# An attention scan's opening: products of the first eight groups split in two, evicted in pairs, and the work around them moved

## The reference

```python
k_n = k / (np.linalg.norm(k, axis=-1, keepdims=True) + 1e-06)
state = np.zeros((B, H, D, D))
for t in range(S):                       # B, H, S, D = 4, 8, 768, 48
    kt, vt, bt = k_n[:, :, t], v[:, :, t], beta[:, :, t, None]
    y[:, :, t] = q[:, :, t] @ state
    state = state + bt * outer(kt, vt - kt @ state)
x = y as (3072 tokens, 384)
h = x @ w_in;  g = (a0 + a1 h + a2 h^2 + a3 h^3) / (1 + |b0| |h| + |b1| h^2 + 1e-06);  x = g @ w_out
h = x @ w2_in; g = relu(h)^2;  out = g @ w2_out          # both 384 -> 2048 -> 384
```

## Time and profile before

| | |
|---|---|
| median of 3 runs (lowest, highest) | 1108.83 us (1108.4, 1108.87) |
| the profiled execution | 1109.15 us, of which the profile's span is 1107.4 us |
| PE, PEld busy | 98%, 85% of the span |
| DVE, ACT, POOL busy | 61%, 59%, 45% |
| granted TensorE clock, mean | 0.997 |
| bytes moved | 74.42 MB, 67 GB/s over the span |

### The profile page before, as it was taken

The page is one execution under the profiler, slowest core; times in us unless marked ns, Lnnn a source line. Parts: engine busy times, 40 slices in busy tenths (PEclk is TensorE's granted clock), DMA queues, the critical chain, the costliest instruction groups (busy, mean ns, idle before and its releaser), DMA issues.

```text
span 1107.4 us, 18346 instructions
## 1 busy us (share of the span) xinstructions
PE 1089.6 (98%) x6370; PEld 940.5 (85%) x6370; DVE 673.2 (61%) x1087; ACT 651.6 (59%) x1277; POOL 502.2 (45%) x807
## 2 busy tenths in 40 slices
PE   8799999999999999999999999999999999999998
PEld 6599999999987888888888888888888888888887
DVE  6976554445459988788887889854343333334332
ACT  5576666555669777877878778653333333333322
POOL 5284888682039878777787778400000000000000
PEclk9999999999999999999999999999999999999999
DMA  9958787566421010100101012140100101010000
GB/s 198 186 103 195 157 180 146 118 148 174 107 73 58 30 57 1 57 1 1 57 1 57 1 44 71 43 129 1 57 1 21 37 1 57 0 57 1 1 29 29
DMA packets 174043, 74.42 MB, mean 67 GB/s; under 512 B 136000, under 2 KB 161728, under 8 KB 172992
## 3 DMA queue, kind: packets, MB, share of 16 engines
q1 hardware_dynamic: 164352, 68.54, 25.5%
q10 hardware_dynamic: 9600, 4.72, 1.8%
HBM read 52.27 MB, written 20.71 MB: 66 GB/s over the span
## 4 chain that ended last, share of the span: by engine, by line
PE 85%; POOL 6%; DVE 4%; issue 2%; SPq 1%; DMA 1%; ACT 0%; ACTq 0%; POOLq 0%
PE ps L1192 12%; PE ps L1194 11%; PE ps L1193 11%; PE ps L1178 11%; PE ps L1180 11%; PE ps L1179 11%; POOL shared L444 3%; POOL scan_x L437 3%; PE ps L548 2%; PE ps L592 2%; PE ps L578 2%; PE ps L595 2%; PE ps L558 2%; PE ps L564 2%; PE ps L525 1%
## 5 line engine op out<-in xcount | busy, mean ns | idle before, releaser
L1178 PE MATMUL ps<-x_split,weights 128*128 128x512 f32 x576 | 224.8, 390 | 1.7 <-DVE g_lo L1337 1.2
L1192 PE MATMUL ps<-g_hi,weights 128*128 128x512 f32 x576 | 224.2, 389 | 0.1
L1180 PE MATMUL ps<-x_split,weights 128*128 128x512 f32 x576 | 224.2, 389 | 0.0
L1179 PE MATMUL ps<-x_split,weights 128*128 128x512 f32 x576 | 224.1, 389 | 0.0
L1193 PE MATMUL ps<-g_lo,weights 128*128 128x512 f32 x576 | 224.1, 389 | 0.0
L1194 PE MATMUL ps<-g_hi,weights 128*128 128x512 f32 x576 | 224.1, 389 | 0.0
L1347 DVE TENSOR_TENSOR common<-common 128x512 f32<-128x512 f32 x96 | 66.4, 692 | 135.0 <-ACT common L1251 133.5
L1257 ACT ACTIVATE g_hi<-common 128x512 fp32r<-128x512 f32 x96 | 60.9, 634 | 141.7 <-PE ps L1194 137.2
L1178 PEld LDWEIGHTS ps<-x_split,weights 128*128 128x128 f32 x576 | 108.1, 188 | 25.2 <-DVE g_lo L1337 2.3
L1410 POOL TENSOR_TENSOR common<-common,g_hi 128x512 f32<-128x512 f32 x96 | 124.2, 1294 | 8.7 <-DVE g_hi L1325 8.7
L1403 POOL TENSOR_TENSOR common<-common 128x512 f32<-128x512 f32 x96 | 124.5, 1297 | 8.0
(11 more groups left out here) (118 smaller groups left out, 1904.5 us busy)
## 6 DMA issues: line engine op xcount, KB each, us to landing
scan_late<-kq_in SPq DMA_DIRECT2D x10, 768.0 KB, 6.5
scan_late<-kq_in SPq DMA_DIRECT2D x16, 384.0 KB, 4.3
shared<-w_in SPq DMA_DIRECT2D x32, 192.0 KB, 2.5
shared<-w_out SPq DMA_DIRECT2D x32, 192.0 KB, 2.6
x_first<-y_t ACTq DMA_DIRECT2D x24, 192.0 KB, 2.7
shared<-x_first SPq DMA_DIRECT2D x6, 768.0 KB, 5.8
x_second<-shared SPq DMA_DIRECT2D x6, 768.0 KB, 4.2
shared<-x_second SPq DMA_DIRECT2D x6, 768.0 KB, 5.9
```

The source lines that it names most:

```text
L1178: pe.matmul(bank(n), lo, x_hi[:, slot, k, :], start=(k == 0), stop=False)
L1179: pe.matmul(bank(n), hi, x_lo[:, slot, k, :], start=False, stop=False)
L1180: mm = pe.matmul(bank(n), hi, x_hi[:, slot, k, :], start=False, stop=(k == KT - 1))
L1192: pe.matmul(ps_y[m], lo, g_hi[:, d, :], start=(f == 0), stop=False)
```

## The change

Six edits. (1) For groups 0 to 7 TensorE makes N alone (`first_n(g)`, a moving operand of 64 columns), and after all eight it makes P (`first_p(g)`, again 64 columns, with the same stationary operand loaded anew, each after `n_first` and after the queries' own load `first_q_loaded`). (2) DVE takes N of two groups in one go (`take_first_pair`: three instructions of 64 x 256 elements for two groups); the eight PSUM banks become one tensor so that an access can span two of them. (3) `load_first` loads only keys, in halves of the former size; the queries of quads 0 and 1 follow in two loads of their own. (4) `k_diag` gets two more slots (`k_diag_aside`, memory that the state uses later), so `spread_keys(2)` and `(3)` wait for no products; `spread_keys(4)` and `(5)` move to behind the second and the fourth `copy_products`, which now waits for `np_done`. A second place for squares (`k_sq_aside`) lets quads 2 and 3 be squared without the wait for the sum just before. (5) The scaling of v of quad 0 by its norms moves from one POOL instruction (L458) to 16 ACT activations of 48 columns, placed behind `squares(4)`. (6) In SP's steps, `load_k(h)` for h >= 9 moves ahead of `store_n`.

```diff
+        z_room = late.take(8 * PAIRS * D)
+        k_sq_aside = z_room[:, 0:QP * D].rearrange("p (q d) -> p q d", q=QP)
+        k_diag_aside = common.ap[0:D2, common.at:common.at + 16 * PAIRS * BL].rearrange(
+            "r (s g f h t) -> r s g f h t", s=2, g=2, h=2, t=BL)
...
+        def squares_of(h):
+            return k_sq_aside if h in (1, 3) else k_sq
+        def diag_of(j):
+            return k_diag_aside[:, j - 2] if j in (2, 3) else k_diag[:, j % 2]
...
-                sp.dma_start(kq[:, j // 2, :, pair], kq_in[:, j // 2, :, pair]).then_inc(first_loaded[j], 16)
+                sp.dma_start(kq[:, j // 2, 0, pair], kq_in[:, j // 2, 0, pair]).then_inc(first_loaded[j], 16)
+            def load_first_q(h):
+                sp.dma_start(kq[:, h, 1], kq_in[:, h, 1]).then_inc(first_q_loaded[h], 16)
...
+            for h in range(2):
+                load_first_q(h)
             load_kq_aside(2)
...
+                for h in range(9, QUADS):
+                    if n == 4 * h - 26:
+                        load_k(h)
                 for h in range(4, QUADS):
                     if n == step_of_quad(h):
                         store_n(h)
...
-                for h in range(8, QUADS):
-                    if n == 4 * h - 26:
-                        load_k(h)
+                if n == 4 * 8 - 26:
+                    load_k(8)
...
-            scale_first_v()        # POOL
...
+            def first_n(g):
+                pe.wait_ge(k_diag_ready, g // 2 + 1)
+                keys_loaded(pe, g // 2)
+                for p in range(PAIRS):
+                    mm = pe.matmul(np_bank(g)[:, p, 0:C],
+                                   diag_of(g // 2)[:, g % 2, 2 * p:2 * p + 2].rearrange("r f h t -> r (f h t)"),
+                                   keys_of(g // 4)[:, 0, g % 4 * PAIRS + p, :], start=True, stop=True)
+                mm.then_inc(n_done, 1)
+            def first_p(g):
+                pe.wait_ge(n_first, g + 1)
+                pe.wait_ge(first_q_loaded[g // 4], 16)
+                for p in range(PAIRS):
+                    mm = pe.matmul(np_bank(g)[:, p, C:2 * C],
+                                   diag_of(g // 2)[:, g % 2, 2 * p:2 * p + 2].rearrange("r f h t -> r (f h t)"),
+                                   keys_of(g // 4)[:, 1, g % 4 * PAIRS + p, :], start=True, stop=True)
+                mm.then_inc(np_done, 1)
...
-            for g in range(UPFRONT):
+            for g in range(FIRST):
+                first_n(g)
+            for g in range(FIRST):
+                first_p(g)
+            for g in range(FIRST, UPFRONT):
                 products(g)
...
-                if h > 0:
+                if h in (2, 3):
+                    act.wait_ge(sum_ready, h - 1)
+                elif h > 3:
                     act.wait_ge(sum_ready, h)
...
-                if j >= 2:
-                    act.wait_ge(np_done, 2 * j - 2)
+                if j >= 4:
+                    act.wait_ge(np_done, 2 * j - (6 if j < 6 else 2))
...
+            def scale_first_v():
+                act.wait_ge(v_loaded[0], 16)
+                values = ring(0)[:, :, :, 0:D].rearrange("r g p d -> r (g p) d")
+                for q in range(QP):
+                    mm = act.activation(values[:, q, :], values[:, q, :], ACT.Copy, scale=norm[:, q:q + 1])
+                mm.then_inc(v_by_act, 1)
             def copy_products(g):
-                if g < FIRST:
-                    act.wait_ge(n_first, g + 1)
+                act.wait_ge(np_done, g + 1)
...
             for g in range(FIRST):
                 copy_products(g)
-            spread_keys(4)
-            spread_keys(5)
+                if g in (1, 3):
+                    spread_keys(4 + g // 2)
...
             squares(4)
+            scale_first_v()
...
+            def take_first_pair(g):
+                h, at = g // 4, g * PAIRS
+                dve.wait_ge(n_done, g + 2)
+                dve.wait_ge(scale_ready, 1)
+                both = ps[:, g * PAIRS * 2 * C:(g + 2) * PAIRS * 2 * C].rearrange("r (q c) -> r q c", c=2 * C)
+                mine = n_all[:, h, g % 4 * PAIRS:(g % 4 + 2) * PAIRS, :]
+                by = key_beta[:, at:at + 2 * PAIRS].unsqueeze(2)
+                later, earlier = slice(0, H2), slice(H2, P)
+                shape = [H2, 2 * PAIRS, BL]
+                dve.tensor_tensor(mine[later, :, 0:BL], both[later, :, 0:BL], by[later].to_broadcast(shape), ALU.mult)
+                dve.tensor_tensor(mine[earlier, :, 0:BL], both[earlier, :, BL:C], by[earlier].to_broadcast(shape),
+                                  ALU.mult)
+                dve.tensor_tensor(mine[earlier, :, BL:C], both[earlier, :, 0:BL], by[earlier].to_broadcast(shape),
+                                  ALU.mult).then_inc(n_first, 2)
...
-            for g in range(FIRST):
-                take_first_n(g)
+            for g in range(0, FIRST, 2):
+                take_first_pair(g)
             turn_blocks()
```

More of the change, by code:

```diff
@@ L125, in build_attention @@
         iq = late.take(8 * PAIRS * (D + C), D2).rearrange("r (g p c) -> r g p c", g=8, p=PAIRS)
-        z_diag = late.take(8 * PAIRS * D).rearrange("p (s q t h d) -> p s q t h d", s=2, q=PAIRS, t=2, h=2)
+        z_room = late.take(8 * PAIRS * D)
+        z_diag = z_room.rearrange("p (s q t h d) -> p s q t h d", s=2, q=PAIRS, t=2, h=2)
+        k_sq_aside = z_room[:, 0:QP * D].rearrange("p (q d) -> p q d", q=QP)
         norm_work = second_x.take(20 * QP).rearrange("p (i q) -> p i q", i=5)
@@ L155, in build_attention @@
         first_loaded = [sem(f"first_loaded{i}") for i in range(4)]
+        first_q_loaded = [sem(f"first_q_loaded{i}") for i in range(2)]
         aside_loaded = [sem(f"aside_loaded{i}") for i in range(2)]
@@ L164, in build_attention @@
         v_ready = sem("v_ready")
-        v_by_pool = sem("v_by_pool")
+        v_by_act = sem("v_by_act")
         k_diag_ready = sem("k_diag_ready")
+        n_done = sem("n_done")
         np_done = sem("np_done")
@@ L678, in spread_keys @@
                 keys_loaded(act, j)
-                if j >= 2:
-                    act.wait_ge(np_done, 2 * j - 2)
+                if j >= 4:
+                    act.wait_ge(np_done, 2 * j - (6 if j < 6 else 2))
                 keys = keys_of(h)[:, 0, i * PAIRS:(i + 2) * PAIRS].rearrange("r (g p) (f t) -> r g (p f) t", g=2, f=2)
                 if 0 in halves:
-                    act.activation(k_diag[:, j % 2, :, :, 0, :], keys, ACT.Copy, scale=own_half[:, 0:1])
+                    act.activation(diag_of(j)[:, :, :, 0, :], keys, ACT.Copy, scale=own_half[:, 0:1])
                 if 1 in halves:
-                    act.activation(k_diag[:, j % 2, :, :, 1, :], keys, ACT.Copy,
+                    act.activation(diag_of(j)[:, :, :, 1, :], keys, ACT.Copy,
                                    scale=own_half[:, 1:2]).then_inc(k_diag_ready, 1)
+            def scale_first_v():
[4 more added lines that the diff above has]
+                mm.then_inc(v_by_act, 1)
             def copy_products(g):
-                if g < FIRST:
-                    act.wait_ge(n_first, g + 1)
+                act.wait_ge(np_done, g + 1)
                 act.activation(group(g)[:, :, D2:D2 + C], np_bank(g)[:, :, C:2 * C], ACT.Copy).then_inc(p_copied, 1)
@@ L878, in take_first_n @@
                 by = key_beta[:, at:at + PAIRS].unsqueeze(2)
[L879 to L890, removed]
+                dve.tensor_tensor(mine, np_bank(g)[:, :, 0:C], by.to_broadcast([P, PAIRS, C]),
+                                  ALU.mult).then_inc(n_first, 1)
             def take_products(g):
@@ L1467, in build_program @@
         memory["g_lo"] = sb(whole, "g_lo", 3 * TN, F32R)
-        banks = [whole.enter_context(nc.psum_tensor(f"ps{i}", [P, PAIRS * 2 * C], F32))[:, :] for i in range(8)]
+        ps = whole.enter_context(nc.psum_tensor("ps", [P, 8 * PAIRS * 2 * C], F32))[:, :]
+        banks = [ps[:, i * PAIRS * 2 * C:(i + 1) * PAIRS * 2 * C] for i in range(8)]
         ff = build_feed_forward(nc, whole, rows, w_in, w_out, moe_coef, memory, banks, x_first, x_second, out)
-        build_attention(nc, dims, memory, banks, kq_in, k_in, v_in, beta_in, blocks, inverse, cross, ff, x_first)
+        build_attention(nc, dims, memory, ps, banks, kq_in, k_in, v_in, beta_in, blocks, inverse, cross, ff, x_first)
 def kernel(q, k, v, beta, moe_w_in, moe_w_out, moe_a, moe_b, moe2_w_in, moe2_w_out):
```

16 lines of the change are left out of this document (5 added, 11 removed).

## The result

The changed kernel takes 1121.55 us (median of 4 runs, 1120.96 to 1122.94), the one before 1108.85 in the same set of runs (4 runs, 1108.4 to 1110.12). The ratio is 1.0114, 95% interval 1.0102 to 1.0126. I had forecast 1108.6 with a range up to 1110.2, so the prediction was wrong: 13 us too low and outside its range. The profiled execution took 1122.94 us with a span of 1120.6, 13.2 more than the span of before; the mean granted clock was 0.988 instead of 0.997.

The account below looks back on a forecast made before the run. It took the opening up to the first steps, then TensorE's own work, as the bound; +0.7 - 0.92 = -0.2 us on the profiled 1109.15 gave 1108.95, as a median 1108.6 us, range 1105.6 to 1110.2 (8 in 10).

Parts of the forecast that it names:

- the first price of the sum: TensorE's split products, groups 0 to 7: 64 moving columns cost 0.86 us a group; N ends at 21.66, P at 28.54.
- The prediction's own sign of being wrong: Wrong in sign if first_n takes half a microsecond or over one a group, or take_n(15) ends under a microsecond later.
- My bounds: TensorE's cost per group of 64-column matmuls: 0.45 us by moving columns alone, 1.29 if short matmuls hide no next weight load.
- The rule: SP's loads landing s late: TensorE loses s - 2.0 once s is over 1.5, gains 1.1 if under 1.0.
- Pairs: DVE's evictions: a pair costs 1.22 us against 1.66 for two groups; the last ends at 22.9 against 22.80, +0.1.
- v off POOL: DVE's second subtraction gains -1.19 us; 16 ACT activations cost 0.22 us each, with more than 4 us left.
- Squares and slots: Opening: squares, key slots and halved first loads bring nothing, since TensorE's products start when the 18 warm-up matmuls end.
- load_k ahead: SP's queue: keys of squares(10) land some 5 us sooner, TensorE's step gains -0.92 us; bounds 0 and -0.92.
- Sum: Whole kernel: +0.7 (late v(2) holding products(17)) - 0.92 = -0.2 us, giving 1108.6 us.
- rival B: TensorE's matmuls cost by moving columns: N done at 18.4, P at 21.5, loads not late; 1105.8 us, chance 0.10.
- D: TensorE's short matmuls hide no weight load, 1.29 us a group; 1115.2 us, decides from 1.0 a group; chance 0.07.
- C: SP's train of loads isn't late (under 1.0 us), so 1.1 + 0.92 come through; 1106.8 us, chance 0.18.

Follow-up runs that it names:

- wide_both: Changed kernel with the 64-column matmuls of both first_n and first_p made 128 columns wide (keys twice, queries twice); 1112.7 us, ratio 1.003.
- short_before: Kernel before, with the products of groups 0 to 7 moving the 64 columns of keys alone, work left out; 1111.62 us, ratio 1.0021.
- wide_n: Changed kernel with only N's matmuls (first_n) made 128 columns wide, P's left at 64; 1114.96 us, ratio 1.0052.
- wide_p: Changed kernel with only P's matmuls (first_p) made 128 columns wide, N's left at 64; 1115.27 us, ratio 1.0052.
- v_early: Changed kernel with load_v(1) and load_v(2) issued ahead of store_n(2); 1116.27 us, ratio 1.0063.
- experiment 7: Also called `both`: kernel before with v of quad 0 scaled on ACT and load_k(h), h from 9, ahead of store_n; 1107.92 us, ratio 0.9984.
- v_on_act: Kernel before with v of quad 0 scaled by 16 ACT activations behind squares(4) instead of one POOL instruction; 1108.37 us, ratio 0.9991.
- v_early_less_warm: Changed kernel with load_v(1) and load_v(2) early and 10 of 17 warm-up matmuls ahead of step 0 left out; 1116.11 us, ratio 1.0063.

## Why the prediction was wrong, step by step

**The step that failed** is the first price of the sum: "So 64 moving columns should cost 0.86 a group ... I take 0.86, the row with the same stationary width." The pace was right for the first four groups (0.88) and in wide_both (0.89). It was wrong by a factor of two in P (1.71), because the clock did not stay where all rows were taken. N was done at 25.1 instead of 21.66, P at 38.75 instead of 28.54; 0.62 of both is that the products began later (15.40 against 14.78 in the chain). The prediction's own sign of being wrong came: first_n took over one microsecond a group (9.69 / 8 = 1.21). My bounds did not hold the price either: 1.29 was the highest at one clock level, and the prediction asks nowhere what the split does to the clock. The profile of before had a warning, since the clock fell in this very stage:

```profile
22.00:25.00 3.00, 0.54 (x4) 0.54 (x5) 2.92 (x5) 2.49 (x6) 0.00 (x0) 1.00 0.96 152
25.00:28.00 3.00, 3.00 (x17) 3.00 (x16) 2.76 (x8) 1.59 (x7) 2.48 (x22) 0.51 0.41 68
```

There an idle stretch of TensorE stands ahead of it. That none is needed, no row of before shows; short_before, wide_n and wide_p, against wide_both, show that the clock fell with TensorE full, under short matmuls.

**What followed from it held.** The rule "with the train late by s, TensorE loses s - 2.0 once s is over 1.5" was worked out for s = 2.7. The trace gives s = 54.96 - 40.51 = 14.45, and products(17) is 12.52 late; the rule says 12.45. In wide_both s = 5.1 and it is 3.0 late (3.1), in wide_n 8.4 and 6.6 (6.4), in wide_p 9.4 and 7.1 (7.4). The chain is the one that I named: take_n(8) at 40.60 instead of 29.6 (10.2 from P, the other 0.8 because products(8) too ran at half clock), another 0.78 in which take_n(9) waited for its products, then SP's queue, v(2), take_products(16). v_early shows the same by taking v out of it. The rule had no term for the clock after the wait (+1.62).

**Pairs:** the last one took 26.37 - 25.14 = 1.23 us, forecast 1.22; right, and against whole products of single groups that is a loss of 0.4 (experiment 7). **v off POOL:** the 58-element subtraction 0.22 us, v_on_act -1.18; right. 16 activations on ACT cost 3.82 us, 0.24 each, forecast 0.22. The 4 us of room that I gave them were not left: ACT came to them at 53.11, and it placed the inverse blocks at 56.71, 4.1 us after the transpose back had ended (50.48 + 2.09 = 52.57). They were hidden all the same, because TensorE's warm-up matmuls ahead of step 0 ran to 60.3. **Squares and slots:** scale_ready came at 15.04 against 15.27, and TensorE did not wait for either; right. **load_k ahead:** -0.92 in the changed kernel as forecast, but v_on_act shows that the stall also goes without it, and `both` that load_k ahead adds nothing to it, so the size was right, and that load_k was the cause is not shown. In the changed kernel the two edits stand together, and no run takes load_k back alone; which of them removed the stall there stays open. **Sum:** -1.19 and -0.92 had the right size, +0.7 should have been +14.1 (12.45 and 1.62 from the measured s, where the 1.1 is already in the rule), and 14.1 - 0.9 = 13.2. Two figures are slips without effect: rival B has P done at 21.5, but 16 groups of 0.45 us from 14.78 on end at 21.98; and the six transfers of store_n(8) took more than a microsecond each at the end (the last two 3.48 us together), so load_k(10) stood 5.7 us behind them.

**The rivals.** D, with a chance of 0.07, had the sign and the path, and the point from which it decides (s = 5.1) was passed. Its mechanism was wrong: no weight load came uncovered (0.88 us a group at full clock). B and C are excluded by 0.88 and by the late train. No rival of mine had two levels of the clock in it, so that D had the sign is luck.

## What to carry over

Price an instruction at both clock levels as soon as a change makes TensorE's instructions smaller or rarer, even where it stays busy 100%: a half-size matmul saved nothing here (0.88 against 0.89 us a group) and then cost double. Where transfers stand in one queue behind a stage, write down how late each may be before an engine asks for it; once that slack (2 us here) was used up, the local loss became one for the whole kernel, one for one, and the same place in the queue bounded the gains until v(2) was loaded earlier. Warm-up matmuls taken from in front of a wait may only be exchanged for a slower clock behind it, so look at the rows behind the wait before counting the gain. And two edits that remove the same stall count once.

## What the runs showed of the hardware that I had not expected

The granted clock fell with TensorE busy 100% by the profile in four kernels with 64-column matmuls against 128-column stationary operands. The short matmuls began, and the first microsecond with a clock below 1.00 lay, at:

| kernel | short matmuls from, to | first below 1.00 | at 0.50 |
|---|---|---|---|
| changed | 15.24, 38.5 | 19 to 20 (0.75) | 20 to 43 |
| short_before | 15.19, 25.1 | 19 to 20 (0.70) | 20 to 33 |
| wide_n | 22.62, 32.4 | 26 to 27 (0.90) | 27 to 37 |
| wide_p | 14.46, 24.8 | 17 to 18 (0.97) | 18 to 31 |
| wide_both | none | none before products(17) | none |

(In short_before TensorE is full up to 25.1 us and idle for 2.5 us behind it, so only the first five microseconds of its low clock lie under short matmuls.) Adding columns to them made the kernel 8.9 us faster (wide_both), leaving columns out of the kernel before made it slower (short_before, ratio 1.0021). That short matmuls are the cause is shown by these five. No run tries a width between 64 and 128 columns here. The Trainium skill, "TensorE: Matmul & The Clock Gate", section "Part 1: The HAM clock gate (the "warmup" mystery)", ties the low clock to an idle TensorE and the high one to a busy one. The stretches of before agree (0.51 behind an idle one). The rows of these four kernels, busy 100% at 0.50, don't if the profile's busy share is the measure, and for this share the measurement decides; whether the page's "busy" means something that this share doesn't show, no run here tells.

The start of the products varied from profile to profile though warm-up and loads ahead of it were the same program: 15.24, 16.02, 15.47, 14.46, 16.01 and 15.47 us in the six kernels with the changed opening. The order is that of the changed kernel, wide_both, wide_n, wide_p, v_early and v_early_less_warm. This spread of 1.6 us is as large as most gains here, and is why differences inside one trace (32.31 against 33.49) say more than the medians.
